# The first of two chained networks in two phases: its up products for all tokens first, its middle result kept in DRAM, and its down product in seven block products for eight over pairs of chunks

## The reference

```
# q, k, v: (8, 8, 576, 64): batch, heads, sequence, head width
q_s = exp(q - max(q, -1));  q_s /= sum(q_s, -1) + 1e-9
k_s = exp(k - max(k, 2));   k_s /= sum(k_s, 2) + 1e-9      # over the sequence
kv  = einsum('bhsd,bhse->bhde', k_s, v)
x   = einsum('bhsd,bhde->bhse', q_s, kv) -> (4608, 512)     # tokens, width
# first network, 512 -> 2048 -> 512
h = x @ w_in
g = maximum(h, 0) + alpha * minimum(h, 0)
y = g @ w_out
# second network, 512 -> 1024 -> 512
h = y @ w_in2
e = exp(h - max(h, -1));  solu = h * e / (sum(e, -1) + 1e-9)
ln = (solu - mean(solu)) / sqrt(var(solu) + 1e-6) * g_ln
out = ln @ w_out2
```

## Time and profile before

| | us |
|---|---|
| median of three runs (1276.09 to 1276.9) | 1276.8 |
| the profiled execution | 1276.15 |
| its span, first to last instruction | 1274.3 |
| PE busy | 1260.3 |
| DVE busy | 709.6 |
| ACT busy | 387.3 |
| POOL busy | 346.2 |

### The profile page before, as it was taken

One profiled execution on the slowest core, in us unless ns is written; L12 is line 12 of the kernel. 1 busy time (PEld: TensorE's weight loads), 2 busy tenths in 40 slices (PEclk: granted clock), 3 DMA queues, 4 the chain that ended last, 5 costly groups with the idle time before them and its releaser, 6 DMA issues.

```text
span 1274.3 us, 16844 instructions
## 1 busy us (share of the span) xinstructions
PE 1260.3 (99%) x6181; PEld 1035.7 (81%) x6181; DVE 709.6 (56%) x989; ACT 387.3 (30%) x625; POOL 346.2 (27%) x289
## 2 busy tenths in 40 slices
PE   7999999999999999999999999999999999999998
PEld 6788887887887887887887888888888888888887
DVE  7865645645645745645745323346755555555553
ACT  4333212212212212212222212124544444444432
POOL 5333233233233233233233222223111111111110
PEclk8999999999999999999999999999999999999999
DMA  8532313313313313313312101210644444444432
GB/s 207 141 120 70 101 38 113 98 37 111 99 37 110 100 37 108 102 37 108 103 37 70 67 1 69 64 67 29 206 155 147 148 142 138 148 147 141 148 124 75
DMA packets 151569, 127.41 MB, mean 100 GB/s; under 512 B 58584, under 2 KB 131824, under 8 KB 150640
## 3 DMA queue, kind: packets, MB, share of 16 engines
q1 hardware_dynamic: 151488, 126.96, 33.0%
q10 hardware_dynamic: 48, 0.01, 0.0%
HBM read 82.33 MB, written 44.61 MB: 100 GB/s over the span
## 4 chain that ended last, share of the span: by engine, by line
PE 97%; DVE 2%; ACT 0%; issue 0%; DMA 0%; POOL 0%; DVEq 0%
PE ps_h L1262 10%; PE ps_h L1264 10%; PE ps_h L1263 10%; PE ps_y L1278 10%; PE ps_y L1279 10%; PE ps_y L1280 10%; PE ps_y L1403 5%; PE ps_y L1404 5%; PE ps_y L1402 5%; PE ps_m L1329 3%; PE ps_h L1329 3%; PE ps_h L1333 3%; PE ps_m L1333 3%; PE ps_h L1328 3%; PE ps_m L1328 3%; PE ps_m L1188 2%
## 5 line engine op out<-in xcount | busy, mean ns | idle before, releaser
L560 POOL TENSOR_TENSOR gl<-tg,gh 128x512 fp32r<-128x512 f32 x144 | 192.7, 1338 | 580.3 <-ACT gh L686 580.3
L686 ACT ACTIVATE gh<-tg 128x512 fp32r<-128x512 f32 x144 | 91.0, 632 | 592.7 <-PE ps_y L1280 427.5
L998 DVE TENSOR_SCALAR tg<-ps_h,acols 128x512 f32<-128x512 f32 x144 | 107.7, 748 | 235.5 <-PE ps_h L1264 233.7
L1262 PE MATMUL ps_h<-xh,W 128*128 128x512 f32 x576 | 227.2, 394 | 0.1
L1264 PE MATMUL ps_h<-xh,W 128*128 128x512 f32 x576 | 224.8, 390 | 0.0
L1263 PE MATMUL ps_h<-xl,W 128*128 128x512 f32 x576 | 224.6, 390 | 0.0
L1278 PE MATMUL ps_y<-gh,WO 128*128 128x512 f32 x576 | 224.6, 390 | 0.0
L1279 PE MATMUL ps_y<-gl,WO 128*128 128x512 f32 x576 | 224.5, 390 | 0.0
L1280 PE MATMUL ps_y<-gh,WO 128*128 128x512 f32 x576 | 224.5, 390 | 0.0
L1262 PEld LDWEIGHTS ps_h<-xh,W 128*128 128x128 f32 x576 | 108.2, 188 | 23.7 <-DVE W L989 0.5
L1264 PEld LDWEIGHTS ps_h<-xh,W 128*128 128x128 f32 x576 | 108.2, 188 | 22.8
(11 more groups left out here) (166 smaller groups left out, 1633.5 us busy)
## 6 DMA issues: line engine op xcount, KB each, us to landing
z_scratch<-zb SPq DMA_DIRECT2D x35, 512.0 KB, 2.6
zt<-z_scratch SPq DMA_DIRECT2D x140, 128.0 KB, 3.0
y_scratch<-stage SPq DMA_DIRECT2D x36, 256.0 KB, 3.7
A<-k_dram SPq DMA_DIRECT2D x16, 512.0 KB, 4.9
V<-v_dram SPq DMA_DIRECT2D x32, 256.0 KB, 4.7
out_dram<-ost SPq DMA_DIRECT2D x32, 256.0 KB, 2.3
A<-q_dram SPq DMA_DIRECT2D x14, 512.0 KB, 4.9
stage<-kx_scratch SPq DMA_DIRECT2D x6, 1024.0 KB, 4.4
```

The source lines that it names most:

```text
L560: nc.gpsimd.tensor_tensor(gl[:, f % 2, :], tg[:, f % 2, :], gh[:, f % 2, :].bitcast(F32), ALU.subtract).then_inc(gl_ok, 1)
L998: nc.vector.tensor_scalar(tg[:, f % 2, :], ps_h[:, f % 2, :], 0.0, slope[:, f:f + 1], ALU.min, ALU.mult).then_inc(t_ok, 1)
L1262: nc.tensor.matmul(o, W1[:, f, 0, a, :], xh[:, a, :], start=(a == 0), stop=False)
```

## The change

The first network is done in two phases.

First phase, chunks 0 to 8: only the up products, which now write all four banks of ps_y in turn. `negative` on ACT takes relu(-h) from PSUM and `prelu` on DVE adds it, scaled by 1 - alpha, to h in a single operation; the result g stays one fp32 tile in one of three buffers (gst) and SP stores it to DRAM (`store_g`, 16 stores of 256 KB for a chunk). The preparation of attention stands in the same kind of list, at other tiles, with buffers of its own (K, Q, QN, kb, qz instead of shared ones), and the chunk loops are written out in full on every engine.

Second phase: chunks 0 and 1, 2 and 3, 4 and 5, 6 and 7 are pairs, and y of a pair is a product of a 2x2 block matrix of w_out (inner width in halves of 8 tiles, output width in halves of 256) by a 2x2 block matrix of g (inner width by chunk of the pair). It is made from seven block products for eight, in the form with 4 sums of g and 4 sums of the weights ahead, and 7 additions behind. Chunk 8 is done the same way, its 512 tokens as two halves of 256. Each block product of a pair is 48 matmuls by 512 columns (four units of 12); of chunk 8 it is 48 matmuls by 256 columns (two units of 24). So 4 x 336 matmuls by 512 columns and 336 by 256 stand where 1728 by 512 stood. ACT and DVE split every unit's right side into high and low (`b_high`, `b_low`, 128x1024 each) and DVE makes the sums (`b_turn`, also 128x1024) and the additions behind (`post`, 128x512). The weights of the second network are split in chunk 8's block products and in the first two tiles of the second network.

On SP, the store of g and the list of a chunk in the first phase:

```diff
+            def store_g(c, f):
+                n = NF * c + f
+                sp.wait_ge(g_ok, n + 1)
+                sp.dma_start(g_dram[c, f, :, :], gst[:, n % 3, :]).then_inc(g_st[n % 3], 16)
...
+            for c in range(B - 1):
+                b = c + 1
+                for f in range(NF):
+                    if c == 0 and f + 4 < NF:
+                        load_w(f + 4)
+                    if f > 0:
+                        store_g(c, f - 1)
+                    if f == 3:
+                        store_kx(b)
+                    if f == 4:
+                        load_kb(b)
+                    if f == 9 and b + 1 < B:
+                        load_kv(b + 1)
+                    if f == 10:
+                        if b + 1 < B:
+                            load_q(b + 1)
+                        store_qz(b, 0)
+                    if f == 11:
+                        store_qz(b, 1)
+                    if f == 12:
+                        load_qz(b, 0)
+                        load_qz(b, 1)
+                    if f == 13:
+                        store_xr(b)
+                store_g(c, NF - 1)
...
+            sp.dma_start(xrg[:, :, :], xr_dram.rearrange("p a b s -> p a (b s)")).then_inc(xr_in, 16)
+            for n in range(4):
+                load_wo(n)
+            for f in range(NF):
+                store_g(B - 1, f)
```

The two operations of g, the first on ACT, the second on DVE, and the two that DVE had:

```diff
+            def negative(c, f):
+                n = NF * c + f
+                act.wait_ge(h_done, n + 1)
+                if n >= 3:
+                    act.wait_ge(g_st[n % 3], 16 * (n // 3))
+                nc.scalar.activation(gst[:, n % 3, :], ps_y[:, f % 4, :], ACT.Relu, scale=-1.0).then_inc(n_ok, 1)
...
-                nc.vector.tensor_scalar(tg[:, f % 2, :], ps_h[:, f % 2, :], 0.0, slope[:, f:f + 1],
-                                        ALU.min, ALU.mult).then_inc(t_ok, 1)
-                dve.wait_ge(t_ok, n + 1)
-                nc.vector.scalar_tensor_tensor(tg[:, f % 2, :], ps_h[:, f % 2, :], 0.0, tg[:, f % 2, :],
-                                               ALU.max, ALU.add).then_inc(g_ok, 1)
...
+                dve.wait_ge(n_ok, n + 1)
+                nc.vector.scalar_tensor_tensor(gst[:, n % 3, :], gst[:, n % 3, :], nslope[:, f:f + 1], ps_y[:, f % 4, :],
+                                               ALU.mult, ALU.add).then_inc(g_ok, 1)
```

PE's list of a chunk in the first phase:

```diff
+            for c in range(B - 1):
+                b = c + 1
+                for f in range(NF):
+                    up(c, f)
+                    if f == 8:
+                        kv_product(b)
+                    if f == 10:
+                        qr_transpose(b)
+                    if f == 12:
+                        xr_product(b)
+                    if f == 14:
+                        x_product(b, 0)
+                        x_product(b, 1)
+                    if f == 15:
+                        x_product(b, 2)
+                        x_product(b, 3)
```

The second phase, a unit on ACT, on DVE and on PE (`wo_part` are the weight blocks and their sums, made and split in chunks 7 and 8 of the first phase), and the second network's weights on DVE:

```diff
+            def b_high(t):
...
+                if t.before >= 0:
+                    act.wait_ge(b_used, t.before + 1)
...
+                nc.scalar.activation(t.tile(rh), t.raw(src), ACT.Copy).then_inc(bh_ok, 1)
...
+            for t in UNITS:
+                if t.r >= EARLY:
+                    b_low(t)
+                if t.k in (0, 1, 2, 4):
+                    b_turn(t)
+                if t.j == t.steps - 1:
+                    if t.k == 0 and t.u > 0:
+                        post("c21", t.u - 1)
+                    if t.k == 3:
+                        post("u", t.u)
+                    if t.k == 4:
+                        post("v", t.u)
+                        post("c22", t.u)
+                    if t.k == 6:
+                        post("c12", t.u)
...
+                pe.wait_ge(bl_ok, t.r + 1)
+                hi, lo = t.tile(rh), t.tile(rl)
+                for s in range(t.kt):
...
+                        nc.tensor.matmul(o, WOc[k][:, 0, kt, cols], hi[:, s, :], start=begin, stop=False,
+                                         skip_group_check=more)
+                        nc.tensor.matmul(o, WOc[k][:, 0, kt, cols], lo[:, s, :], start=False, stop=False,
+                                         skip_group_check=more)
+                        mm = nc.tensor.matmul(o, WOc[k][:, 1, kt, cols], hi[:, s, :], start=False, stop=end,
+                                              skip_group_check=more)
...
-                if first and r == 0:
-                    w2_low(7)
+                if first and r < 2:
+                    for f in range(4 * r, 4 * r + 4):
+                        w2_low(f)
```

More of the change, by code:

```diff
@@ new lines, in linear_attention_two_mlps, with number, ends, sums @@
+        UNITS = [Unit(r) for r in range(PAIRS * PARTS * 4 + PARTS * 2)]
+        LAST_U = PAIRS
+        EARLY = 2
+        def number(u, k, j):
+            return u * PARTS * 4 + k * (2 if u == PAIRS else 4) + j
+        def ends(u, k):
+            return number(u, k, (2 if u == PAIRS else 4) - 1) + 1
+        def sums(u, n, j):
+            return u * 16 + n * (2 if u == PAIRS else 4) + j + 1
+        SUM_AT = {1: 0, 2: 1, 3: 2, 6: 3}
+        def by_block(buf):
+            return buf.rearrange("p (i t a) -> p t i a", i=4, t=TT)
@@ L416, in _, with load_wo @@
-            chunk(0, first=True)
-            for c in range(1, B - 1):
-                chunk(c)
-            store_y(B - 2)
-            sp.wait_ge(qn_ok, 3 * B)
-            sp.wait_ge(xr_st, 16 * B)
-            sp.dma_start(A[:, 0:MAIN], xr_dram.rearrange("p a b s -> p (a b s)")).then_inc(xr_in, 16)
+            def load_wo(n):
+                half, cols = ((0, 0), (0, 1), (1, 1), (1, 0))[n]
+                part = (A11, A21, A22, A12)[n]
+                sp.dma_start(part, w_out[half * F1 // 2:(half + 1) * F1 // 2, cols * HM:(cols + 1) * HM]
+                             .rearrange("(f p) n -> p f n", p=P)).then_inc(wo_in[n], 16)
@@ new lines, in _, with p1_copy @@
+            for f in range(NF):
+                if f == NF - 1:
+                    for t in UNITS[:EARLY]:
+                        b_high(t)
+                negative(LAST, f)
+                if f in (5, 9, 13):
+                    wo_high(4 + (5, 9, 13).index(f))
+            def p1_copy(u):
+                n = TOK // 2 if u == PAIRS else TOK
+                act.wait_ge(b_used, ends(u, 0))
+                if u == 0:
+                    act.wait_ge(h_done, NF * NC)
+                else:
+                    act.wait_ge(y22_st, 16 * u)
+                nc.scalar.activation(p1[:, :, 0:n], ps_m[:, :, 0:n], ACT.Copy).then_inc(p1_ok, 1)
@@ L1021, in _ @@
+            q_max(0, 0)
+            k_columns()
+            q_max(0, 1)
+            q_max(0, 2)
+            k_sub(0)
+            q_sum(0, 0)
+            q_sum(0, 1)
+            q_sum(0, 2)
+            kv_norm(0)
+            q_low(0, 0)
+            kv_low(0)
+            for j in range(1, KT):
+                q_low(0, j)
             for j in range(KT):
-                x_low(0, j, first=True)
+                x_low(0, j)
             dve.wait_ge(w_lo, 3)
-            def chunk(c, prepare=True, first=False):
+            dve.wait_ge(acols_ok, 2)
@@ L1408, in tiles @@
                 for r in range(4):
-                    if not (first and r == 0 or last and r == 3):
+                    if not (last and r == 3):
                         m1_product(m + (r + 1) // 4, (r + 1) % 4, first=(first and r < 3))
```

1282 lines of the change are left out of this document (679 added, 603 removed).

## The result

The changed kernel takes 1367.74 us (median of 4, 1366.44 to 1368.89), the kernel before, measured beside it, 1276.55: 1.0716 times as long, 95% interval 1.0703 to 1.0729. The forecast was 1358 us, its range 1296 to 1400.

What follows compares the result with a forecast made beforehand. PE bound the kernel before; its work would fall 43.3 us, but first-phase waits (+79 chunks 1 to 5, +23, +7, +4) and 12 behind add up to +81.7 on 1276.15: 1358 us, 80% range 1296 to 1400.

Steps and rivals of the forecast that it cites:

- the likeliest case: First phase: SP's list, DVE's chain and queued transfers make a middle chunk 68 us for PE's 52.2; 48 in 100.
- step 5: Middle chunk, SP's list: turned q ready at about 38 us, its first store issued behind k, v, q loads at 42.2.
- 7 next chunk: Middle chunk's end: 16 loads of turned q and the work behind take about 16 us, next chunk at 67.3.
- Steps 1 to 4: Middle chunk up to g of tile 8 at 33.4 us, including kb's load and PE's 4 us wait before k by v.
- Step 6: Middle chunk: the first store of turned q queues behind the data of k, v and q and lands at 51.3 us.
- the rule: Transfers: a semaphore write lands only after that DMA engine's earlier writes; store lands at 51.3 us, without it 45.
- the transfers don't queue: Rival on the turned q's store: lands 2.7 us after issue, six chunks 6.3 us shorter, 1320 us; 20 in 100.
- chunk 0: First chunk: 13 low parts of weights on DVE and weights queued behind k, v, q; 75 us, +23 in the sum.
- the stalls behind: Chunk 7 and later: 4 us in chunk 7, 12 for first unit, chunk 8's products and second network's start.
- PE stays the bound: Rival for the first phase: prepared work fits beside PE if turned q is back by 48 us; 1245 us; 9 in 100.
- The clock falls at both idles: Rival for middle chunks: k by v also runs at 1.2 GHz, 3 to 4 us in six chunks, 1380 us; 15 in 100.
- 256 columns cost as 512: Rival for chunk 8's 336 matmuls: 256 columns cost as much as 512, 32 us more, 1390 us; 8 in 100.

Runs made afterwards that it cites:

- after: The changed kernel as described, with no further edit, against the kernel before: 1367.74 us, 1.0716 times as long.
- kb_early: Changed kernel with the store of the small maxima, the load of kb, and DVE's reduction and subtraction of kb one tile earlier: 1337.1 us.
- kept_warm: Changed kernel with 52 unused 128-column matmuls filling PE's two idles in each of chunks 0 to 6: 1372.4 us.
- order_moved: Changed kernel with only SP's list reordered, the next chunk's loads of k, q and v moved away from the turned q: 1337.2 us.
- kvq_small: Changed kernel with the same list, but from batch 2 on each load of k, v and q brings only one head: 1330.5 us.
- loads_spread: Changed kernel with q turned on PE, kb earlier, chunk 7's g stores before w_out, second-network weights split earlier, k/q/v loads spread between g stores: 1270.4 us.
- pe_turn: Changed kernel with q turned by 16 PE transposes a chunk instead of through DVE and DRAM: 1327.9 us.
- all_four: Changed kernel with q turned on PE, kb loaded earlier, chunk 7's g stores ahead of w_out's loads, second network's weights split earlier: 1296.2 us.

## Why the prediction came out right

**The mechanism** was that of the likeliest case: PE gives up the bound in the first phase to the order in SP's list and the chain over DVE. Of the signs named for it these are there: k by v 65 to 70 us apart (68.0 to 69.4), its wait of about 4 us released by ACT's exponential (4.0 to 4.6), a granted clock below 1 in every middle chunk, and a pair of chunks in the second phase at 76.6 us (four took 306.4) for 76.2. One is there in one chunk of five only: a store issued over 3 us after DVE has written it (step 5).

**Step by step**, with time 0 at 245.48 us of the trace of after:

| step | forecast | measured |
|---|---|---|
| 1 g of tile 3 | 13.7 | 13.5 |
| 2 kb lands | 18.8 | 19.8 |
| 2 k subtracted | 26.7 | 27.2 |
| 3 PE's wait before k by v | 4 | 4.06 |
| 4 g of tile 8 | 33.4 | 33.3 |
| 5 turned q ready, first pair | 38 | 43.1 |
| 5 first store of it issued | 42.2 | 45.0 |
| 6 it lands | 51.3 | 53.2 |
| 7 next chunk | 67.3, with the clock 68 | 68.9 |

Steps 1 to 4 held within 1 us. The load of kb took 5.8 us where I had used 4.4 of the earlier trace rows. Step 5 failed in one of its halves. I said the store would be issued over 3 us after DVE had it ready: it was 1.9 us here, 1.8 to 3.2 in the five middle chunks. Both sides were late. The four loads of v took SP 5.50 us to issue, 2.93 before, and DVE came to turn q at 43 since k by v ran at half clock. kb_early and kept_warm, in which it didn't, show the waiting in SP's list that step 5 is about: 6.4 to 7.4 and 5.8 to 7.0 us. PE's wait at the products of q by kv is 5.8 to 7.6 us, not the 11.5 that follow from the steps, for the same reason: it worked longer at half clock in between. That the chunk came out at 68.9 for 68 is in part luck: the store left 2.8 us later than forecast and landed in 8.2 us for 9.1.

**Step 6 and the rule**: landings of 7.0 to 8.3 us are what I forecast (7 to 9). The Trainium skill's page DMA: Bandwidth & Descriptors (Queues, rings and completion order) has the semaphore write of a transfer land only after every earlier write of that DMA engine. The trace agrees as far as it shows: in the chunk above the store lands at 298.68 us, 1.1 us after the last load of q, which left SP before it. The runs agree as well: 2.6 us with no loads ahead (order_moved, kvq_small), 4.2 to 5.2 on a queue of its own, 7.0 to 8.3 behind the loads. That the bytes ahead cost the time is shown; whether the rule or only their turn on the engines does it, these runs can't tell. The rival "the transfers don't queue" had put 2.7 us on the landing: with the loads ahead that is false. Its price of 6.3 us a chunk is near the 6.1 by which order_moved, which takes the queue away, is shorter on average.

**Where the sum was low**, by 10.3 us: chunk 0 by 2.7, the middle ones by 2.8, chunk 6 by 3.4, the stalls behind by 3.6, the start by 1.2; against it the 256-column matmul at 0.120 us (three from 912.42 to 912.77 in the trace) rather than 0.13, 3.4 us less. 336 x 0.120 are 40.3 us. The weight load of 107 ns that the Trainium skill gives for 128 columns (TensorE: Matmul & The Clock Gate, LDWEIGHTS) agrees with that: it fits within the 0.120, and the estimate made with it was about 40. (The rows of PEld show such a load as 0.19 us, longer than the distance of two; as with matmuls, a row is longer than its turn.) In chunk 7 a store of g behind w_out's loads landed after 11.16 us and PE waited 3.2, near the 4 forecast.

**The rivals.** "PE stays the bound" gave 1245 us and needed the turned q back by 48 us of a chunk; it was there at 58. It describes what the kernel becomes when the lists are put right: middle chunks of 54 us in loads_spread. Of the 46.7 us that the block products save, 24 still go in the first phase there (chunks 0 to 6 take 387.9 us, before 363.7 without the down matmuls; by the 2.2 us a chunk of above, some 15 of the 24 are the transposes that PE took over), 1 at the start and 15 behind, so 6.8 us of the span remain. "The clock falls at both idles" was right as an event (k by v at 5.98 us for 3.52) and wrong in its price of 3 to 4 us a chunk: with most of these falls gone kept_warm is no faster (1372 us for 1368). "256 columns cost as 512" is refuted by the 0.120.

**What stays open.** Of the 19.6 us in chunk 7 and behind, 16.4 are named above. Moving the split of the second network's weights left its two waits at 7.7 us for 8.7; what would cover them was not tried.

## What to carry to other kernels

When work that bounds an engine is taken out of a stretch, walk one period of the rest through every queue in order, SP's issues included, before counting the saving: busy shares (44.5 of 52.2 us on DVE) said it would fit, and it took 68. A wait that is taken away at one place can come back at the next: kb_early took the 4 us before k by v away, and the wait for turned q grew by as much. So judge an edit by the length of the whole period, not by the wait. Here kb_early and pe_turn brought 31 and 40 us alone and 66 together. The same block of loads then delayed something else, first turned q and then the stores of g with their three buffers. Spreading large prefetches between small stores, or more buffers behind these stores, was worth 2% (1296 us to 1270 and 1273). With all these edits the loss of 7% became a gain of 0.5% (interval 0.3 to 0.6%), most of it through the edits before that last one.

## What the runs showed of the hardware

- The granted clock fell to half in the changed kernel at each PE idle of 4.0 to 7.6 us in its middle chunks (k by v in 5.98 us for 3.52). The length of an idle does not tell by itself. Before the first block product PE stood 1.79 us in after and in kb_early alike; the next matmuls then started 0.427 us apart in after, at half clock, and 0.23 in kb_early, at the full one. In one chunk of all_four k by v took 5.47 us behind an idle of 1.88, in another 3.58 behind 1.14. The two rows of after, the two of kb_early, the one of all_four:

```profile
606.41 0.63 PE L1554 MATMUL ps_m<-rl,WOc 128*128 128x512 f32 x1
606.84 0.63 PE L1556 MATMUL ps_m<-rh,WOc 128*128 128x512 f32 x1
```
```profile
575.92 0.39 PE L1554 MATMUL ps_m<-rl,WOc 128*128 128x512 f32 x1
576.15 0.39 PE L1556 MATMUL ps_m<-rh,WOc 128*128 128x512 f32 x1
```
```profile
357.99 5.47 PE L1400 MATMUL ps_m<-V,K 128*64 128x65 f32 x80 [1.88 <-ACT K L724]
```

- What such a fall costs depends on who sets the length: about nothing in after (kept_warm), some 3 us in the chunk of loads_spread that PE bounds.
- Pairs of weight load and matmul in this precision have a distance of 0.2267 us at 512 columns and 0.120 at 256.
- SP's issue of the same four loads of v took 2.8 to 3.3 us in the kernel before, where no transfer was under way (chunks 1 to 6), and 5.4 to 6.1 in the changed one, right behind the loads of k. With few bytes (kvq_small) it took 2.01 in the same place; those loads are smaller themselves, so that run does not part the two.
- A store of 512 KB landed 2.6 us after its issue with no loads ahead, and 7.0 to 8.3 behind those of k, v and q. A second queue let it land some 3 us sooner, and the loads issued next on the first one some 2 us later after their issue.
